# Rows of the MLP stage taken in the order in which the middle stage makes them, its first tiles begun during the middle stage, and 66-row transfers cut in 64 and 2

## The reference, cut to what matters

```python
# x: (4, 4224, 192); every step keeps this shape
x = local_attention(x, weight_gen)              # 7 taps, softmax weights           stage A
mixed = real(fft(fft(x, axis=1), axis=2))       # over all 4224 tokens, 192 channels stages A and B
u  = x + mixed
un = (u - mean(u)) / sqrt(var(u) + 1e-6)        # per token                          stage C
x  = u + relu(un @ w_ch1) @ w_ch2               #                                    stage C
theta = x @ w_theta                             #                                    stage C
zr, zi = x * cos(theta), x * sin(theta)         #                                    stage C
y  = w_tok_r @ zr + w_tok_i @ zi                # tokens mixed, two 4224 x 4224       stage M
u  = x + y
out = u + relu(u @ w_ch)                        #                                    last part of M
```

## Time and profile before

| | us |
|---|---|
| median of 3 runs | 3277.54 (3277.0 to 3280.19) |
| the profiled execution, its own time | 3279.67 |
| its span, first to last instruction | 3277.9 |
| busy: PE, DVE, POOL, ACT | 2985.2, 2592.8, 1579.0, 1299.8 |
| stage A | 0 to 366 |
| stage B, PE's first to last product | 376.5 to 481.5 |
| PE's first MLP product | 506.2 |
| stage C until the first product of M | to 1128, handover to 1143.6 |
| stage M, of which its last chunk | to 3263.7, from 3016.5 |

### The profile page before, as it was taken

The page is one execution under the profiler, slowest core; times in us unless marked ns, Lnnn a source line. Parts: engine busy times, 40 slices in busy tenths (PEclk is TensorE's granted clock), DMA queues, the critical chain, the costliest instruction groups (busy, mean ns, idle before and its releaser), DMA issues.

```text
span 3277.9 us, 57687 instructions
## 1 busy us (share of the span) xinstructions
PE 2985.2 (91%) x17218; PEld 2824.7 (86%) x17218; DVE 2592.8 (79%) x4308; ACT 1299.8 (40%) x2452; POOL 1579.0 (48%) x1527
## 2 busy tenths in 40 slices
PE   3555678999999799999999999999999999999999
PEld 3444327998998799999999999999999999999999
DVE  9999455777777888888878788787878788887776
ACT  1111225666666533333333333333333333333443
POOL 5666204666667644544545354444534454443221
PEclk8777898999999999999999999999999999999999
DMA  6566462323233465565556566565656566655442
GB/s 215 195 212 203 140 253 78 121 97 121 98 121 131 152 223 214 215 224 214 219 209 225 212 219 234 199 230 202 235 197 235 211 221 223 219 218 181 140 138 74
DMA packets 212227, 612.07 MB, mean 187 GB/s; under 512 B 15824, under 2 KB 59152, under 8 KB 212080
## 3 DMA queue, kind: packets, MB, share of 16 engines
q1 hardware_dynamic: 202928, 597.41, 51.0%
q10 hardware_dynamic: 9152, 12.98, 1.4%
HBM read 393.66 MB, written 216.66 MB: 186 GB/s over the span
## 4 chain that ended last, share of the span: by engine, by line
PE 76%; issue 7%; POOLq 6%; DVE 4%; DMA 2%; ACT 2%; DVEq 2%; POOL 1%; ACTq 0%; SPq 0%
PE banks L1502 55%; PE banks L1369 11%; POOLq L988 5%; PE banks L1444 4%; PE banks L1446 2%; DVE zl L749 2%; PE banks L1430 2%; DVEq L797 1%; DMA fraw<-f_low 1%; POOL head L986 1%; ACT zh L1202 1%; PE banks L1581 1%; PE banks L1416 1%; PE banks L1418 1%; DVE wl L744 0%
## 5 line engine op out<-in xcount | busy, mean ns | idle before, releaser
L1502 PE MATMUL banks<-zh,wh 128*128 128x384 f32 x3828 | 1295.3, 338 | 46.4 <-DVE rbuf L801 46.4
L1502 PE MATMUL banks<-zh,wl 128*128 128x384 f32 x3828 | 1281.8, 335 | 0.0
L1502 PE MATMUL banks<-zl,wh 128*128 128x384 f32 x3828 | 1280.9, 335 | 0.0
L801 DVE TENSOR_TENSOR rbuf<-rbuf,banks 128x384 f32<-128x384 f32 x1168 | 642.7, 550 | 254.9 <-PE banks L1502 221.1
L1502 PEld LDWEIGHTS banks<-zh,wh 128*128 128x128 f32 x3828 | 720.1, 188 | 69.5 <-DVE rbuf L801 48.2
L1502 PEld LDWEIGHTS banks<-zl,wh 128*128 128x128 f32 x3828 | 720.5, 188 | 0.0
L1502 PEld LDWEIGHTS banks<-zh,wl 128*128 128x128 f32 x3828 | 719.6, 188 | 0.0
L1020 POOL TENSOR_TENSOR wsum<-wraw 128x384 f32<-128x384 f32 x176 | 179.6, 1020 | 1105.9 <-DVE wl L744 980.4
L1194 ACT ACTIVATE wh<-wsum 128x384 fp32r<-128x384 f32 x704 | 370.3, 526 | 771.0 <-PE banks L1502 729.5
L744 DVE TENSOR_TENSOR wl<-wsum,wh 128x384 fp32r<-128x384 f32 x664 | 504.5, 760 | 40.6 <-ACT wh L1194 16.7
L1194 ACT ACTIVATE wh<-wraw 128x384 fp32r<-128x384 f32 x528 | 278.0, 527 | 498.9 <-PE banks L1502 498.9
(11 more groups left out here) (142 smaller groups left out, 4244.7 us busy)
## 6 DMA issues: line engine op xcount, KB each, us to landing
wraw<-w_pairs SPq DMA_DIRECT2D x176, 768.0 KB, 6.7
rbuf<-y_scr SPq DMA_DIRECT2D x176, 768.0 KB, 5.7
y_scr<-rbuf SPq DMA_DIRECT2D x160, 768.0 KB, 4.0
xin<-x_pad SPq DMA_DIRECT2D x22, 1728.0 KB, 8.2
z_scr<-zsc SPq DMA_DIRECT2D x33, 768.0 KB, 3.9
zraw<-z_scr SPq DMA_DIRECT2D x33, 768.0 KB, 7.4
x_scr<-x1s SPq DMA_DIRECT2D x22, 576.0 KB, 4.9
t_scr<-tst ACTq DMA_DIRECT2D x44, 288.0 KB, 5.0
```

Of the source, the lines that this page charges most:

```text
L801: dve.tensor_tensor(part, part, dst(k, i), ALU.add).then_inc(r_done, 1)
L1502: last = pe.matmul(dst, l[w][:, q, :], r[par][:, operand, q, :], start=starts and q == 0 and t == 0, stop=q == 2 and t == 2, skip_group_ch ...
```

## The change

- `x1_scr`, `m_scr`, the token matrices and `out` take a new row order (`row_order`): MLP tile n < 32 holds exactly what group n of stage B makes (2 `i` x 2 frequencies x 32 values of `a`), and tile 32 holds the rows `a` = 32 of all 128 frequencies. The token matrices are permuted before the launch.
- A tile's `UR` is then loaded in four transfers of 32 rows (SP, L507 of the changed kernel) in place of one of 128, and `out` is stored in four of 32 rows in place of one of 128 for each half tile.
- In stage B the `t_scr` load is cut in 64 and 2 rows (L423). The store becomes 64 rows to one place (L436), one row (L437) and one row with the two parts reversed (L441). The `f_low` load moves from SP to ACT, behind ACT's copy of the group.
- ACT rounds the weights before its first group of stage B, while the last data of stage A travel.
- The last four groups are taken out of the loop on ACT and DVE, and SP, ACT, DVE and POOL do steps -3 to -1 of stage C between them.

```diff
+def row_order():
+    rows = []
+    for n in range(NT - 1):
+        for i in range(2):
+            for w in range(2):
+                rows += [residue(2 * n + i, w) + P * a for a in range(NT - 1)]
+    return np.array(rows + [c + P * (NT - 1) for c in range(P)])
...
             def load_t(j, s):
-                sp.dma_start(traw[s][0:NR].rearrange("p i b d -> p i (b d)"),
-                             t_scr[ds(8 * j + 2 * s, 2)].rearrange("i w n x -> (w n) i x")).then_inc(b_in[s], 16)
+                rows = t_scr[ds(8 * j + 2 * s, 2)].rearrange("i w n x -> (w n) i x")
+                for lo, hi in ((0, 64), (64, NR)):
+                    sp.dma_start(traw[s][lo:hi].rearrange("p i b d -> p i (b d)"), rows[lo:hi]).then_inc(b_in[s], 16)
...
             def load_b(j, s):
                 sp.wait_ge(g_ready, 8 * (j - 1) + 2 * s + 2)
                 load_t(j, s)
-                load_f(j, s)
...
             def store_b(j, s):
+                sp.dma_start(m_scr[ds(gi, 1)].rearrange("o (i q) x -> q (o i) x", i=2), rows[0:64]).then_inc(m_out[s], 16)
+                sp.dma_start(m_scr[NT - 1:NT, ds(2 * gi, 2), :], rows[64:65]).then_inc(m_out[s], 16)
...
+                    sp.dma_start(m_scr[NT - 1:NT, ds(P - 1 - 2 * gi, 2), :], rows[65:66, ::-1]).then_inc(m_out[s], 16)
...
+            def load_u(n, s):
+                wait(sp, u_ready, n)
+                sp.dma_start(mbuf[:], m_scr[ds(n, 1)].rearrange("o p x -> p (o x)")).then_inc(m_in, 16)
+                wait(sp, y_out, 16 * (n - 5))
...
+                for part, c in quarters(n):
+                    sp.dma_start(flat(tile(s))[part], x1_rows[ds(c, 1), 0:32, :].rearrange("o a x -> a (o x)")
+                                 ).then_inc(m_in, 16)
...
-            run_c(step_c, sp)
+            for s in range(4):
+                if s < 3:
+                    sp.wait_ge(m_out[s], 48)
+                    step_c(s - 3, s - 3)
+                store_b(SB - 1, s)
+            for s in range(4):
+                sp.wait_ge(m_out[s], 48 * SB)
+            run_c(step_c, sp, 0)
...
             def store_o(n, h, u, number):
+                for part, c in quarters(n):
+                    sp.dma_start(out_rows[ds(c, 1), 0:32, 2 * h:2 * h + 2].rearrange("o a b d -> a (o b) d"),
+                                 ost[u][part]).then_inc(o_out[u], 16)
...
+            group_b(SB - 1, 0)
+            group_b(SB - 1, 1)
+            step_c(-2, -2)
+            group_b(SB - 1, 2)
+            group_b(SB - 1, 3)
+            step_c(-1, -1)
+            run_c(step_c, dve, 0)
...
+                if more:
+                    act.dma_start(fraw[s][0:NR], f_low[:, ds(8 * (j + 1) + 2 * s, 2), :]).then_inc(b_in[s], 16)
...
+            for s in range(3):
+                group_b(SB - 1, s, False)
+            step_c(-2, -2)
+            group_b(SB - 1, 3, False)
+            step_c(-1, -1)
+            run_c(step_c, act, 0)
...
             def step_c(n, s):
+                if isinstance(n, int) and n == 0:
+                    pe.wait_ge(m_ready, 8 * SB)
...
+                    if isinstance(n, int) and n == -1:
+                        pe.wait_ge(m_ready, 8 * SB - 3)
```

More of the change, by code:

```diff
@@ L92, in fourier_constants @@
             f_low[1, :, i, 1, 1] = -np.sin(p2)
+    f_low = f_low.reshape(2 * NT, P // 2, 2, 2 * NT)
+    f_low = np.concatenate([f_low[..., :NT - 1], f_low[..., NT:2 * NT - 1], f_low[..., NT - 1::NT]], axis=-1)
     none = np.zeros((D2, D))
@@ L97, in fourier_constants, with residue @@
             f_low.reshape(2 * NT, P // 2, 4 * NT).astype(np.float32))
+def row_order():
[5 more added lines that the diff above has]
+    return np.array(rows + [c + P * (NT - 1) for c in range(P)])
+def residue(i, w):
+    if not w:
+        return i
+    return P // 2 if isinstance(i, int) and i == 0 else P - i
 def wait(eng, sem, value):
@@ L289, in preparing, with run_c @@
             return isinstance(n, int) and NT - 3 <= n < NT
-        def run_c(step_of, eng):
-            for n in range(-3, 5):
+        def run_c(step_of, eng, first):
+            for n in range(first, 5):
                 step_of(n, n)
@@ L477, in load_r, with quarters @@
                              y_scr[ds(2 * p, 2)].rearrange("i p x -> p i x")).then_inc(r_in[k], 16)
+            def quarters(n):
+                for i in range(2):
+                    for w in range(2):
+                        q = 2 * i + w
+                        yield slice(32 * q, 32 * q + 32), residue(2 * n + i, w)
+            def load_u(n, s):
+                wait(sp, u_ready, n)
+                sp.dma_start(mbuf[:], m_scr[ds(n, 1)].rearrange("o p x -> p (o x)")).then_inc(m_in, 16)
+                wait(sp, y_out, 16 * (n - 5))
+                if isinstance(n, int) and n == NT - 1:
+                    sp.dma_start(flat(tile(s)), x1_scr[S - P:S]).then_inc(m_in, 16)
+                    sp.sem_inc(m_in, 48)
+                    return
+                for part, c in quarters(n):
+                    sp.dma_start(flat(tile(s))[part], x1_rows[ds(c, 1), 0:32, :].rearrange("o a x -> a (o x)")
+                                 ).then_inc(m_in, 16)
             def step_c(n, s):
                 if live(n + 3):
[L481 to L484, removed]
+                    load_u(n + 3, s + 3)
                 if live(n - 2):
@@ L902, in finish_e @@
                 dve.wait_ge(ep_ready, number)
-                wait(dve, o_out[u], 16 * before)
+                wait(dve, o_out[u], 64 * before)
                 dve.scalar_tensor_tensor(ost[u][:], banks[:, 6 + u % 2, 0:BH].rearrange("p (b d) -> p b d", b=2),
@@ L1155, in _ @@
                 act.activation(hi, raw, ACT.Copy).then_inc(cwh_ready, 1)
-            with act.Fori(1, P // 16) as j:
+            step_b(0)
+            with act.Fori(1, SB - 1) as j:
                 step_b(j)
@@ L1421, in _ @@
             step_b(0)
-            with pe.Fori(1, P // 16) as j:
+            with pe.Fori(1, SB) as j:
                 step_b(j)
```

84 lines of the change are left out of this document (40 added, 44 removed).

## The result

| | kernel before | changed kernel |
|---|---|---|
| median of 14 runs, us | 3277.64 | 3286.53 |
| lowest to highest | 3273.0 to 3281.53 | 3283.76 to 3290.06 |
| ratio, 95% interval | | 1.0027, 1.0019 to 1.0035 |

What follows compares the result with a forecast made beforehand. Stage B was taken as bound by eleven full DMA engines, SP close behind, and the handover by a string of latencies. First product -13.2 and end +1.0 gave -12.2 us, from 3277.54 to 3265, range 3257 to 3274.

Steps and rivals of the forecast that it cites:

- SP's share of a turn: Stage B: SP's issues and register work sum to 2.9 to 3.46 us a turn, taken as 3.2, setting the pace.
- the choice for the last row's issue: Stage B's reversed one-row store: 0.33 to 0.88 us; staying dear was a rival giving 3272, about even odds.
- What SP's pace was before: Stage B before: SP's issues took 2.8 us without a wait, turns 3.25, so SP was close behind the DMA engines.
- The reading of 11.0 closing packets an issue: Stage B: 812 small packets over 74 issues meant 11 engines share a transfer, eleven full and five idle.
- The new limit of the engines: Stage B: 64 rows shared by 16 engines lower the DMA limit from 3.3 us a turn to 2.3 to 3.0.
- T0: SP's first issue for an MLP tile behind its stage B loop: forecast 469.8 us against 486.6, bounds 462.6 to 476.0.
- The first product: PE's first MLP product, behind the handover: forecast at 493.0 us instead of 506.2, 13.2 us gained.
- The string: Handover: latencies from SP's first tile issue to PE's first MLP product, 23.2 us, against 19.6 before.
- Stage C: SP has seven issues a step instead of four: zero cost; 1.35 us a tile, 40 us, if the cover were gone.
- Last chunk: Stage M's last chunk: SP's 16 stores take 9 us more or less of a 17.2 us pair; zero until the end.
- the rival of slow stores (3285): Stage M's last chunk: 32-row stores at 0.88 + 0.2 us cost 20 us; chance 0.06, shared with stage C's loss.
- The end: Stage M's very end: a burst of store issues delays the last store by 0.6 to 2.2 us, taken as 1.0.

Runs made afterwards that it cites:

- e9: Kernel before, with `f_low` issued by ACT behind its copies instead of by SP from the second group on: 3275.3 us, ratio 0.9991.
- e5: Changed kernel, with one load and one store of 66 rows in each turn of stage B: 3273.9 us, ratio 0.9982.
- e8: Changed kernel, with three SP issues a turn, 2-row load on ACT, last two rows stored together, first MLP tile earlier, DVE reordered: 3264.5 us, ratio 0.9957.
- e1: Changed kernel, with stage B's row load as one transfer of 66 rows instead of 64 and 2: 3273.0 us, ratio 0.9987.
- e7: Changed kernel with the 66-row load, first MLP tiles begun only behind stage B's last group on every engine: 3284.4 us, ratio 1.0014.

## Why the prediction was wrong

**The step that failed** is SP's share of a turn: "each issue from the loop costs 0.53 to 0.58", the 64-row issues priced like the 66-row one beside them. Measured from start to start: load of 64 rows 0.88 (I had 0.54), 2 rows 0.49 (0.54), store of 64 rows 0.86 (0.58), one row 0.55 (0.58), the reversed row 0.98 (0.59 to 1.14, taken as 0.87), branch 0.09 (0.08). In all 3.85 for 3.2, of which 0.62 are the two 64-row issues. Even my upper bound, 3.46, was too low. A row that I had read showed the price: the 64-row issues of L1118 at 602 to 772 ns. I used it for ScalarE and not for the issues of the same height on SP. The bound had to come from it, and 3.46 + 0.6 would have been 4.1 us a turn. That SP would set the pace was right, and so was the choice for the last row's issue (0.71 us, between my 0.33 and 0.88).

**What SP's pace was before.** The change took away an `f_low` issue that I counted as part of SP's pace. SP wasn't the pace (e9), the transfers on eleven engines were, as I had it (3.3 us read, 3.24 estimated from the transfers alone, 3.23 to 3.28 in e9 and e5). The reading of 11.0 closing packets an issue fits both. The new limit of the engines came out less well: 2.3 to 3.0 predicted, 2.59 for the transfers alone without `f_low`, but 3.06 in the kernel (e8), just above my range. So even with SP out of the way the split was worth some 0.2 us a turn, not 0.3 to 1.0; I had taken 23.3 KB/us an engine to hold with sixteen of them, and e8 moves 280 GB/s with all sixteen full, 17.5 on each. The change lifted the old limit a little and put SP's in its place, 0.6 us above the old one.

**T0** was to be 393 + 24 x 3.2 = 469.8, and was 395.7 + 24 x 3.86 = 488.4: 15.8 us by the pace, 2.7 by the start, where I had expected the moved weight rounding to gain 1 us and SP's loop began later instead. With the load in one piece (e1) T0 was 471.1.

The first product came 17.6 us later than forecast (510.6 for 493.0): 18.6 of it is T0's, less 1.0 in the string.

**The string** from T0 was 22.2 us for 23.2 predicted. It was near only because of the late T0: with T0 at 471 it is 25.7, for the queue ahead of the tile's loads, of which I had allowed 0.6 us and which is 4.0 (9.2 against 5.2). The overlap itself is worth 11.4 us (e7).

**Stage C** zero, as predicted: 621.5 us from the first product to stage M's preparation against 621.8, with PE as busy. **Last chunk** zero, as predicted: 247.20 us of PE in both, pairs of 17.18. SP's 32-row stores cost a median of 0.32, less than the 0.37 I had, and the rival of slow stores (3285) met the time by chance, not by its mechanism. **The end**: +1.0 predicted, 3286.9 - 2942.9 against 3277.9 - 2935.0 is +1.1.

**The rival that was missing** is the plain one: more issues on the one engine that issues them all, at the price of the nearest row of the same shape. The condition that I named for being wrong, turns over 3.5 us, was the right one to watch.

## What to carry to other kernels

Splitting a transfer so that more DMA engines share it lifts the engines' limit, here by 0.2 us a turn, and adds to the issuing engine's: write both as us a turn, issue by issue from start to start, and price each issue by a row of the same number of rows and pieces, not by its neighbour. If an engine issues all the time and shows no wait, moving one issue to another engine tells in one run whether it is the pace. An early start of the next stage is worth less than the time by which it starts early (16.8 us at T0 were 11.7 at the first product), since its first loads queue behind the stage that still runs; load what is ready long before the end.

## What was unexpected in the hardware

- An issue of exactly 64 rows costs 0.60 us against 0.28 for 63 and 0.30 for 66 (two pieces of 3072 bytes a row), on SP and ScalarE, for loads and stores, and 0.65 in the busy kernel. Of the 18 numbers of rows tried no other has a median over 0.38, apart from one row of two pieces (0.56). Why isn't settled.
- The number of rows also decides how long a transfer takes alone, and steeply. The issues of the six loads of 60 rows, then of 61, each load with a store of as many rows behind it:

```profile
L26 SPq DMA_DIRECT2D buf<-x x6: 330/330/337, 213.9 to 248.0; - x6
L26 SPq DMA_DIRECT2D buf<-x x6: 232/233/233, 254.9 to 418.5; - x6
```

From one load to the next it takes (248.0 - 213.9)/5 = 6.8 us with 60 rows and (418.5 - 254.9)/5 = 32.7 us with 61, for one load and one store.
- With nothing else on the chip, loads of 64 rows move 207 GB/s with all engines full, and loads of 66 rows 203 with eleven. Together with stores the 64 rows are ahead, 360 against 270.
